# One TensorE step moved ahead of another at the start of a fused attention, channel-mix and gated-convolution kernel

## The reference

```python
# 1 attention: heads 0-3 see the last 32 positions, heads 4-7 every 32nd position
scores = scale * q @ k.T ; scores = where(mask[h], scores, -1e9)
attn = softmax(scores) ; x = attn @ v              # x: (4, 576, 512)
# 2 channel mix
x_prev = x shifted by one position (zero first)
xk = mu_k * x + (1 - mu_k) * x_prev ; xr = mu_r * x + (1 - mu_r) * x_prev
k = max(xk @ w_k, 0) ; v = (k * k) @ w_v           # w_k: 512 x 1024, w_v: 1024 x 512
r = sigmoid(xr @ w_r) ; x = r * v
# 3 gated convolution
h = max(x @ w_in, 0) ; c = convolution of h over 3 positions ; out = (h * sigmoid(c)) @ w_out
```

## Time and profile before

| | us |
|---|---|
| median of 3 runs | 527.5 |
| lowest and highest run | 527.18, 527.78 |
| the profiled execution | 526.82 |
| span of its trace, first to last instruction | 525.0 |
| TensorE busy in the span | 516.4 |

### The profile page before, as it was taken

The page is one execution under the profiler, slowest core; times in us unless marked ns, Lnnn a source line. Parts: engine busy times, 40 slices in busy tenths (PEclk is TensorE's granted clock), DMA queues, the critical chain, the costliest instruction groups (busy, mean ns, idle before and its releaser), DMA issues.

```text
span 525.0 us, 15350 instructions
## 1 busy us (share of the span) xinstructions
PE 516.4 (98%) x6202; PEld 478.9 (91%) x6202; DVE 322.9 (62%) x812; ACT 287.5 (55%) x783; POOL 114.6 (22%) x139
## 2 busy tenths in 40 slices
PE   8799999999999999999999999999999999999997
PEld 6578999999999999999999999988998899889985
DVE  5769986657657566657644745881497039707910
ACT  4389288296394592690880815751583057416720
POOL 8039972031021040140221791000000000000000
PEclk9999999999999999999999999999999999999999
DMA  9893323334243342341106136001301130010011
GB/s 194 204 278 56 72 78 62 64 91 66 68 92 62 91 69 47 82 68 41 49 2 252 45 88 210 2 0 61 110 1 32 49 110 0 35 46 0 0 40 60
DMA packets 98772, 39.07 MB, mean 74 GB/s; under 512 B 91156, under 2 KB 91284, under 8 KB 98708
## 3 DMA queue, kind: packets, MB, share of 16 engines
q1 hardware_dynamic: 94334, 33.16, 25.6%
q0 software_dynamic: 1632, 4.36, 2.5%
q10 hardware_dynamic: 2742, 0.66, 0.8%
HBM read 28.72 MB, written 9.44 MB: 73 GB/s over the span
## 4 chain that ended last, share of the span: by engine, by line
PE 98%; DVE 1%; issue 0%; ACT 0%; POOL 0%; DVEq 0%; POOLq 0%
PE ps L805 19%; PE ps L815 19%; PE ps L697 9%; PE ps L698 9%; PE ps L699 8%; PE ps L748 7%; PE ps L749 7%; PE ps L750 6%; PE ps L683 5%; PE ps L560 3%; PE ps L622 2%; PE ps L603 2%; PE ps L756 1%; PE ps L672 0%; PE ps L657 0%
## 5 line engine op out<-in xcount | busy, mean ns | idle before, releaser
L496 POOL TENSOR_TENSOR k_lo<-k,k_hi 128x288 fp32r<-128x288 f32 x64 | 59.4, 932 | 192.6 <-ACT k_hi L877 192.5
L1292 DVE SCALAR_TENSOR_TENSOR cbuf<-hbuf,cols_c,cbuf 128x576 f32<-128x576 f32 x64 | 52.4, 818 | 63.5 <-ACT cbuf L982 62.4
L748 PE MATMUL ps<-k_hi,wb_hi 128*128 128x288 f32 x256 | 76.1, 297 | 0.0
L749 PE MATMUL ps<-k_lo,wb_hi 128*128 128x288 f32 x256 | 75.5, 295 | 0.0
L750 PE MATMUL ps<-k_hi,wb_lo 128*128 128x288 f32 x256 | 75.5, 295 | 0.0
L697 PE MATMUL ps<-xk_hi,wa_hi 128*128 128x288 f32 x224 | 67.0, 299 | 0.0
L698 PE MATMUL ps<-xk_lo,wa_hi 128*128 128x288 f32 x224 | 66.1, 295 | 0.0
L699 PE MATMUL ps<-xk_hi,wa_lo 128*128 128x288 f32 x224 | 66.1, 295 | 0.0
L815 PE MATMUL ps<-wb_hi,g_hi 128*128 128x512 f32 x144 | 57.5, 399 | 0.0
L815 PE MATMUL ps<-wb_hi,g_lo 128*128 128x512 f32 x144 | 56.7, 394 | 0.0
L815 PE MATMUL ps<-wb_lo,g_hi 128*128 128x512 f32 x144 | 56.5, 392 | 0.0
(11 more groups left out here) (112 smaller groups left out, 1160.3 us busy)
## 6 DMA issues: line engine op xcount, KB each, us to landing
x2d<-x2s SPq DMA_DIRECT2D x8, 576.0 KB, 3.1
x2raw<-x2d SPq DMA_DIRECT2D x4, 1152.0 KB, 5.8
out_dram<-ob SPq DMA_DIRECT2D x16, 256.0 KB, 2.0
raw<-in_q_dram SPq DMA_DIRECT2D x96, 36.0 KB, 1.9
raw<-in_k_dram SPq DMA_DIRECT2D x96, 36.0 KB, 1.9
wk_raw<-in_moe_w_k_dram SPq DMA_DIRECT2D x4, 512.0 KB, 9.4
wv_raw<-in_moe_w_v_dram SPq DMA_DIRECT2D x4, 512.0 KB, 5.1
ws<-in_moe_w_in_dram POOLq DMA_DIRECT2D x4, 512.0 KB, 7.3
```

Of the source, the lines that this page charges most:

```text
L496: nc.gpsimd.tensor_tensor(k2_lo[:, m], k2[:, m % K2RING], k2_hi[:, m].bitcast(F32), ALU.subtract).then_inc(k2_done, 1)
L748: nc.tensor.matmul(dst, wb_hi[:, f, cols], k2_hi[:, f, :], start=(f == 0), stop=False)
L749: nc.tensor.matmul(dst, wb_hi[:, f, cols], k2_lo[:, f, :], start=False, stop=False)
L1292: nc.vector.scalar_tensor_tensor(out=c, in0=h[:, o:o + S], scalar=conv[:, o, m:m + 1], in1=c, op0=ALU.mult, op1=ALU.add).then_inc(conv_ste ...
```

## The change

The second group of early w_k products (channel tile 1, output tiles 0 to 3) is put ahead of the values of half 0's strided block in TensorE's order. All instructions and all waits stay as they are, and the other engines' orders too.

```diff
             keep_warm(WARM_SLOT)
             for m in range(EARLY_M):
                 plain_w_k(m, (0,))
-            values(0, 2)
             for m in range(EARLY_M):
                 plain_w_k(m, range(1, EARLY_T))
+            values(0, 2)
 
             for h in range(NH):
                 for slot in range(SLOTS):
```

## The result

| | before | changed |
|---|---|---|
| median, us | 527.68 | 529.69 |
| lowest to highest | 525.96 to 530.57 | 528.32 to 532.72 |
| executions | 20 | 20 |

The ratio is 1.0041, with a 95% interval from 1.0029 to 1.0053: the change makes the kernel 2.2 us slower by the ratio, 2.0 by the medians. I had forecast 1.1 us slower. The direction is right and the size is half of what was measured; 529.69 lies within 0.01 us of my upper end.

The account below looks back on a forecast made before the run. TensorE, busy 516.4 of 525.0 us, was taken as the bound, with no slack from values to the fourth tile's product. +1.17 - 0.08 = +1.09 us on 527.5 gave 528.6 us, range 527.6 to 529.7.

Parts of the forecast that it names:

- steps 1 to 4: Moved w_k products delay the strided values to 22.98 us and the fourth mixed tile's product to 26.66: +1.17 us.
- the old wait: 1.14 us hole ahead of the strided values (L622), ended by the last six vs DMAs landing a little before 21.78 us.
- three signs: Fourth tile's matmul starts before 26.3 us, L622 still waits after the moved products, or the end is not about as late.
- step 5: At half 1's local values (L603), a shorter wait for DMA vl gives back 0.08 us, bounds 0 and 0.47.
- The sum of +1.09: Whole kernel: +1.17 us of delay at the early products less 0.08 at vl, giving 528.6 us; chance 0.72.
- the clock: Rival: behind the new idle time some 3 us of TensorE work at half rate lose about 1.5 us, 530.1; chance 0.07.
- late landing: Rival: vs lands so late that both orders wait, 527.5 us; chance 0.17 together with the delay being made up later.
- filled hole: Rival: ready work fills the 1.14 us hole before the strided values, up to 1.14 us faster, 526.4; chance 0.04.

Follow-up runs that it names:

- set 1: One of three sets of runs, each on one chip beside the kernel before; at clock 1.00 the changed kernel took 526.4 us against 525.4.
- set 3: Another of the three sets of runs, with its own row of the kernel before, whose median at clock 1.00 was 525.7 us.
- set 2: Another of the three sets of runs, with its own row of the kernel before, whose median at clock 1.00 was 526.7 us.
- the zeros: Changed kernel plus 15 zero matmuls of 224 columns in the 1.67 us hole behind the strided values, run twice; median 529.07 us in the first run.
- the four profiles named above: Profiles with zero matmuls added, two products moved, vs transfers early, or four warm-up matmuls left out; in all the clock falls at 17.0 to 17.3 us.

## Why the prediction was half right

**The cover of the early products (steps 1 to 4): right.** Values at 22.98 forecast, 23.02 measured in an execution that is 0.04 late; third tile's product 25.73 and 25.78; fourth's 26.66 and 26.71; transposes 27.2 and 27.27; hole 1.67 and 1.67. That the chain behind the values has no slack is shown by the profiles: from the start of the values to the transposes it takes 4.24 to 4.26 us in all eleven in which the 88 value matmuls run as in the kernel before, whether the values start at 20.66 or at 24.76. The dose agrees with it, within its noise: two products moved cost 0.2 us at full clock, four cost 1.0. None of the three signs that I had named for being wrong came about.

**What ends the old wait: right for its start, incomplete.** `vs` held the first matmul (its last update at 21.72, the weight load at 21.78). The packet with the instructions for the 25th ended at 20.12; by the 1.5 to 1.6 us that lie between the two elsewhere they were due at about 21.7 too, which the profile of before could not show because the first wait covered it. I argued that the landing can't wander by much more than the 0.60 us between three runs. That was wrong: in the nine profiles with these transfers in their old place it is from 21.04 to 22.89 us.

**The 0.08 us given back at `vl` (step 5): not found at clock 1.00.** There the weight load of L603 still waits for `vl`, 1.21 us later than before, and 0.02 us are given back. I took SP's schedule as fixed. In that execution `vl` was issued from 28.65 us, not 27.61, and its last landed at 40.60, against 39.39; half of the 1.0 us was there at 21.2 us, before the changed order could act. Over the profiles with `vl` on SP's queue its first issue is from 27.41 to 30.10 us. In the profile with the slow clock, where TensorE comes 1.6 us later still, the wait for `vl` is gone and 0.1 us is given back.

**The sum of +1.09 at clock 1.00: right,** +1.0 by the medians of set 1 and +1.1 between the two profiled executions at clock 1.00.

**The step that failed is the clock: the sum put it at nothing and the rival got 0.07.** What is missing in +1.09 is about 1 us of falls. I wrote that the granted clock would be "1.00 all along", because the profiled execution of the kernel before had kept 1.00 through its 1.14 us hole. That was one execution: of 99 others 33 had less than 1.00. The price was right (some 1.5 us forecast, 1.5 measured between the two profiles), its frequency was not: 17 of 32, against 12 of 35 of the kernel before beside it. With the medians of set 1, the heaps add 3/12 x 1.5 + 3/12 x 3.4 = 1.2 us to the mean of the changed kernel and 12/35 x 0.5 = 0.2 to that of before. With the 1.0 of the order that makes 2.0; the mean spans of set 1 are 527.6 and 525.7, 1.9 apart. The 0.5 for a fall in the kernel before is a figure of set 1 only: it is 0.7 in set 3, and -0.7 in set 2. I should have weighed the clock as part of the sum and not as a rival. The Trainium skill's advice against idle gaps between bursts of matmuls ("TensorE: Matmul & The Clock Gate", section "Why this matters for your kernels") is given there for gaps longer than the 1.67 us of this change, so by its letter it did not make this change worse, though I wrote that it did. The measurement goes further than the page here: the fall from 27.88 us stands behind a gap that is shorter.

That a fall costs more in the changed kernel than in the one before (1.5 us against 0.5 for 0.997, in set 1) fits where the profiled one lies: at 27.9 to 31.3 us, in dense work. It is not the whole account of the heaps, since with the zeros, too, the heap at 0.997 is 1.2 and 2.2 us above that at 1.00, and the fall profiled there lies at 16.97 us. Between the two profiles with zeros the values start 1.56 us apart, and 1.43 of that were there at the last warm-up matmul at 14 to 16 us, ahead of the fall: such executions are late by their start and the longer wait for instructions, and the fall itself adds 0.1. In the kernel before part of such a delay can vanish in the wait for `vs`, which the changed kernel no longer has. That is argued: no profile of the kernel before with a fall was taken, and that its falls lie at 17 us, as in the four profiles named above, is likely but not shown.

**The other rivals.** The late landing and the filled hole did not come about in the profiles. Filling idle time gained nothing since the work put in had been covering a chain elsewhere.

## What to carry to other kernels

Before ready work is moved into a hole, ask what it covers where it stands: here four products hid a chain of copying and mixing, and moving them exchanged a hole of 1.14 us for one of 1.67 us further on. Where an order opens a hole ahead of dense matmuls, price a fall of TensorE's clock by its frequency, and take that from many executions with their clocks, since one profile at 1.00 says nothing of it. Waits put down to "issue" in a stream of tiny matmuls can be for the instructions themselves: see whether they keep their place in the stream when instructions are added ahead. And before a fall of the clock is put down to a hole, look whether it begins behind that hole: in the kernel without the four warm-up matmuls it had begun 2 us ahead of it.

## What the runs showed of the hardware

- The same hole of 1.67 us was followed by a granted clock of 0.50 in one profiled execution and not in another, with the same instructions at the same times to 0.13 us from 18.5 us on. The fall from 27.88 to 31.29 us, in dense work, cost 1.5 us.
- TensorE stood 0.4 to 2.4 us for instructions early in the kernel, until 1.2 to 1.8 us after a packet of 16 KB on the instruction queue had ended. The place is fixed by the number of instructions ahead: 48 more moved it by 24 weight load and matmul pairs.
- With fifteen zero matmuls added to an open sum, in 1.61 us of a hole, none of 24 executions had a second fall of the clock, against 8 of 32 without.
- From a DMA's last semaphore update to the weight load that had waited for it there were 0.06 us in three profiles (`vs_head`) and 0.04 in four (`vl`).
